# Attention scores as one 64-row product per head, into two PSUM banks, in place of one 128-row product with zero blocks

## What is computed

```
scores = scale * q @ k^T                        # per batch and head, 576 x 576
Dmat   = gamma_h ** (i - j)  where i >= j, else 0
x      = (scores * Dmat) @ v
```

## Time and profile before

| | |
|---|---|
| median of 3 runs | 727.16 us (726.26 to 732.09) |
| the profiled execution's own time | 731.02 us |
| its span, first to last instruction | 729.2 us |
| TensorE matmul busy | 669.4 us (92%), 4248 instructions |
| VectorE, ScalarE, GpSimd busy | 282.0, 220.0, 363.3 us |
| attention stage | 11.9 to 153.8 us |
| score product (L613) | 192 instructions, 50.5 us busy |

### The profile page before, as it was taken

How to read it: one execution, slowest core, us unless ns; L and a number is a source line. 1 busy time by engine, 2 the same in 40 slices (tenths; PEclk the granted TensorE clock), 3 DMA queues, 4 the chain that set the end, 5 groups by cost and what they waited for, 6 DMA issues and landing times.

```text
span 729.2 us, 14483 instructions
## 1 busy us (share of the span) xinstructions
PE 669.4 (92%) x4248; PEld 549.5 (75%) x4249; DVE 282.0 (39%) x595; ACT 220.0 (30%) x505; POOL 363.3 (50%) x226
## 2 busy tenths in 40 slices
PE   2989799953999699999999999978999999999997
PEld 1667467732778588888888888856998998898895
DVE  2456456666112233222324233334375066057031
ACT  1445355420212122222222222234434244244211
POOL 2646436404355999999999998938011002000000
PEclk9999989985899899999999999988999999999999
DMA  9999959513994434334444334332102102100101
GB/s 248 271 229 264 265 136 268 147 33 29 102 345 147 133 137 151 136 131 146 144 130 142 131 130 143 92 117 68 37 19 77 36 0 79 50 0 0 65 1 66
DMA packets 69717, 88.34 MB, mean 121 GB/s; under 512 B 14592, under 2 KB 42880, under 8 KB 69568
## 3 DMA queue, kind: packets, MB, share of 16 engines
q1 hardware_dynamic: 51264, 64.40, 30.4%
q0 software_dynamic: 3472, 11.28, 6.5%
q10 hardware_dynamic: 14944, 12.24, 5.2%
HBM read 71.89 MB, written 17.84 MB: 123 GB/s over the span
## 4 chain that ended last, share of the span: by engine, by line
PE 80%; DMA 9%; issue 4%; DVE 3%; POOL 2%; ACT 1%; POOLq 0%; ACTq 0%; DVEq 0%
PE ps L721 25%; PE ps L711 24%; DMA xg<-x_rows,slot_token 5%; PE ps L654 5%; PE ps L613 4%; PE ps L624 3%; PE ps L709 2%; PE ps L712 2%; PE ps L642 2%; PE ps L755 2%; PE ps L637 2%; PE ps L718 2%; DMA consts_sb<-constants 2%; PE ps L722 2%; DMA x_rows<-x_sb 1%
## 5 line engine op out<-in xcount | busy, mean ns | idle before, releaser
L542 POOL TENSOR_TENSOR w_lo<-stage,w_hi 128x1024 f32 x48 | 115.6, 2408 | 8.0 <-POOL w_hi L540 8.0
L540 POOL TENSOR_TENSOR w_hi<-stage,zero 128x1024 f32 x48 | 92.6, 1930 | 5.6 <-issue 5.6
L711 PE MATMUL ps<-w_lo,w_hi 128*128 128x288 f32 (+2 forms) x268 | 93.0, 347 | 0.0
L496 POOL TENSOR_TENSOR q_blocks<-q_in,consts_sb 64x576 f32<-64x576 f32 x32 | 44.8, 1401 | 70.7 <-PE ps L642 57.1
L721 PE MATMUL ps<-w_lo,xt_hi 128*128 x184 | 73.8, 401 | 0.3 <-issue 0.3
L721 PE MATMUL ps<-w_lo,ht_hi 128*128 x184 | 72.3, 393 | 0.0
L711 PE MATMUL ps<-w_hi,w_lo 128*128 128x512 f32 (+2 forms) x201 | 69.9, 348 | 0.0
L711 PE MATMUL ps<-w_hi 128*128 128x512 f32 (+2 forms) x201 | 69.8, 347 | 0.0
L1258 DVE TENSOR_TENSOR xt_lo<-ps,xt_hi 128x512 fp32r<-128x512 f32 x25 | 17.3, 691 | 126.0 <-ACT xt_hi L964 116.6
L977 ACT CAST ht_hi<-ps 128x512 fp32r<-128x512 f32 x50 | 26.9, 591 | 126.8 <-PE ps L755 117.0
L721 PE MATMUL ps<-w_hi,ht_hi 128*128 x161 | 63.2, 392 | 0.0
(11 more groups left out here) (177 smaller groups left out, 1452.4 us busy)
## 6 DMA issues: line engine op xcount, KB each, us to landing
stage<-in_w SPq DMA_DIRECT2D x64, 512.0 KB
y_slots<-y_sb ACTq DMA_DIRECT2D x25, 256.0 KB
q_in<-in_q_t SPq DMA_DIRECT2D x16, 288.0 KB, 3.6
kn_in<-in_k_n SPq DMA_DIRECT2D x16, 288.0 KB, 4.5
k_in<-in_k_t SPq DMA_DIRECT2D x16, 288.0 KB, 4.8
v_in<-in_v_n SPq DMA_DIRECT2D x16, 288.0 KB, 6.1
x_rows<-x_sb ACTq DMA_DIRECT2D x16, 288.0 KB, 4.4
out<-out_sb SPq DMA_DIRECT2D x16, 256.0 KB, 2.0
```

What stands on the lines that cost most here:

```text
L496: nc.gpsimd.tensor_tensor(q_blocks[d, u, h, :].rearrange("p (c t) -> p c t", c=NC), q_in[d, u, :].rearrange("p (c t) -> p c t", c=NC), q_d ...
L540: nc.gpsimd.tensor_tensor(hi, stage[:, j % HP, :], zero[:, 0:1].broadcast_to([P, PIECE]), ALU.add).then_inc(hi_done, 1)
L542: nc.gpsimd.tensor_tensor(lo, stage[:, j % HP, :], hi.bitcast(F32), ALU.subtract).then_inc(split_done, 1)
L711: nc.tensor.matmul(to, *p, start=False, stop=False)
```

## The change

The score product is made per head: only the head's 64 rows of `k_in` and of its plane in `q_blocks`, 96 columns each. Head 0 and head 1 write to two different banks, (0, 1) for even chunks and (6, 7) for odd ones, so there are two score buffers in place of three, and `scores` wait for the mask of c-2. The sum of the state moves from bank 6 to bank 2. The zero blocks stay, since L637 still reads them.

```diff
-        score_ps = ps[0:C, 0:3, 0:2 * C]
+        def score_ps(k):
+            low = (0, 6)[k]
+            return ps[0:C, low:low + 2, 0:C]
...
-        state_ps = ps[:, 6, 0:DH]
+        state_ps = ps[:, 2, 0:DH]
...
-                u, k = hp % 2, c % 3
+                u, k = hp % 2, c % 2
...
-                pe.wait_ge(probs_ready, n * NC + c + 1)
-                nc.tensor.matmul(score_ps[:, k, :], k_in[:, hp, c * C:(c + 1) * C],
-                                 q_blocks[:, u, :, c * C:(c + 1) * C]).then_inc(scores_ready, 1)
+                pe.wait_ge(probs_ready, n * NC + c + 2)
+                t = slice(c * C, (c + 1) * C)
+                for h, d in enumerate(heads):
+                    mm = nc.tensor.matmul(score_ps(k)[:, h, :], k_in[d, hp, t], q_blocks[d, u, h, t])
+                mm.then_inc(scores_ready, 1)
...
-                nc.vector.tensor_tensor(probs[:, c % 3, :, :], score_ps[:, c % 3, :].rearrange("p (h t) -> p h t", h=2),
+                nc.vector.tensor_tensor(probs[:, c % 3, :, :], score_ps(c % 2),
                                         inside_c[:, 2 * hp:2 * hp + 2, :], ALU.mult).then_inc(probs_ready, 1)
```

## The result

The changed kernel takes **809.92 us** (808.36 to 810.47, 4 runs) against 729.54 us before on the same chips (726.26 to 732.09, 4 runs): ratio **1.110**, 95% interval 1.104 to 1.116. I had forecast 729.1 us, with a range up to 746. The profiled execution took 809.8 us with a span of 808.0 us. The last turn product of the attention starts at 232.4 us in place of 153.8: 78.6 of the 78.8 us that the span grew lie in the attention stage.

A forecast was written before the change was run, and what follows sets the result against it. TensorE's queue was taken to bound the attention stage; 75 x 0.02 at full clock + 0.5 + 0.2 at loop starts - 5 x 0.07 in cold steps = +1.9 us, rounded to 2, on 727.16: 729.1 us, range 723 to 746.

The forecast's parts named there:

- (4): Score part of a step at the lower clock: 0.70 us against 0.77, -0.07 us on some 9 steps.
- forecast case: Whole kernel: row halves work in parallel, switch and open load cancel the saving, clock rises as before; 729.1 us, chance 72.
- rival (C): Attention steps: thinner streaming doesn't earn the full clock, +1.0 us a step; 770 or 807 us, chance 8 in 100.
- (1): Score products: 96 columns per head, both row halves at once, two pairs taking 0.17 us in place of 0.326.
- Rival (A): Score products: the heads' halves run one after the other, +17 us, 745 us; chance 12 in 100.
- (2): Before the scores: one more change of array shape, from 128 to 64 rows, costing 0.09 us of emptying a step.
- (3): Score weight load: no longer hidden under the product before, 0.08 us, two heads' loads starting some 0.01 us apart.
- Rival (B): Before the scores: no emptying between 128-row and 64-row arrays, load and switch hidden; 722 us, chance 6 in 100.
- (5): Two score buffers: the tighter mask wait costs nothing in steady steps, 0.5 and 0.2 us at the loop starts.
- (6): The rest: mask reading two banks, moved state, one more matmul a step and later stages add nothing.

The follow-up runs named there:

- warmed kernel: Changed kernel plus unread dense products in each loop pass, 18 before the first scores and 22 before those of c=2: 741.50 us, ratio 1.0175.
- hybrid: Changed kernel with the scores of the first 12 of 48 steps per loop pass as one 128-row, 192-column product: 733.42 us, ratio 1.0065.
- early-only: Changed kernel plus 36 unread dense products ahead of the loop, none inside it: 776.01 us, and 810.59 us in the second run.
- two-buffer kernel: Kernel before with only the score buffers cut from three to two, scores waiting for the mask of c-2: 733.17 us, ratio 1.0043.

## Why the prediction was wrong

**The step that failed is (4), carried into the choice between the forecast case and rival (C).** In (4) I counted some 9 steps at the lower clock, the same as before the change, with no row that says that the changed steps would earn the higher one; the runs show all 96 at it. What (4) says of one such step was right (2.32 us in place of 2.39). The price of (C) was right (2.32 us a step and 807 us; measured 2.32 and 809.9), its chance of 8 in 100 was not, and the range left it out. The argument against it was that the clock had fallen only after TensorE stood idle and never for thin streaming. That row is about *keeping* the level; I used it for *getting* it. The runs separate the two: the warmed kernel and the hybrid (dense first steps) keep the full clock through thin steps (1.345 us each), the changed kernel and, in its profiled run, the second pass of the early-only one (dense products ahead of the loop) never get it in 96 and 48 of them. Which part of the changed step withholds it, fewer columns, the added change of shape or the row halves in short pieces, the runs don't separate. The earlier trace rows also held the question: in the kernel before every rise came while it worked at the lower clock in steps of the dense form.

**(1) Half the columns, both halves at once: right.** Two pairs at the full clock take what four column halves take: in the warmed kernel two of the four instructions start at 109.75 and two 0.16 us later. Rival (A) fell; its price was added up a little high (0.18 x 75 is 13.5, the sum 744 us).

**(2) and (3) One more emptying and an open load: right.** 0.44 us forecast, 0.44 measured in the warmed kernel, +0.016 a step. The open load shows by itself in the two-buffer kernel: from 61.79 to 62.29 are 0.50 us, so 0.08 are left for it beside 0.33 of streaming and 0.09 of emptying. Rival (B) fell with the warmed kernel's rows. So even at full clock the halved product gives nothing: 0.16 us less streaming against 0.17 us of switch and load.

**(5) The tighter wait: right where it stood, and its condition too.** In the warmed changed kernel the step two after c = 4 takes the 1.345 us of the others; without the emptying, in the two-buffer kernel, the wait lay bare at 0.15 us once in six steps. The loop start, in the changed kernel:

```profile
126.03 0.67 DVE L1091 TENSOR_TENSOR probs<-ps,consts_sb 96x192 f32<-96x192 f32 x2 [3.09 <-PE ps L620]
126.43 0.40 PEld L620 LDWEIGHTS ps<-q_blocks,k_in 64*96 64x96 f32 x4 [0.47 <-DVE probs L1091]
...
127.00 0.29 PEld L631 LDWEIGHTS ps<-v_in,k_dec 96*64 96x64 f32 x4 [0.17 <-issue]
...
127.17 0.34 PEld L649 LDWEIGHTS ps<-probs,v_in 96*64 96x64 f32 x4
127.27 0.53 PE L649 MATMUL ps<-probs,v_in 96*64 96x96 f32 x4
```

The first mask ends at 126.38 and the output product starts at 127.27, 0.89 us later, where it was 0.06: +0.83, forecast 0.8.

**(6)** held for VectorE and ScalarE, which wait for TensorE as before. The hybrid, 4.7 us (3.1 to 6.5 us by its interval) over the kernel beside it, is dearer than my 2 us for the form at full clock: 72 x 0.016 = 1.2 and two starts of up to 0.8 leave some 2 us. A term that (6) left out may be in it: TensorE's jump back to the top of the loop.

```profile
88.95 2.45 PE L624 MATMUL ps<-q_blocks,k_in 128*96 128x192 f32 x6 [8.27 <-issue]
```

TensorE stood 8.27 us there, where it was 0.29 in the kernel before, and the pause from turn product to turn product was 13.8 us against 9.3.

## What to carry to other kernels

Before you shorten a product in a stretch where TensorE is the bound, ask whether the steps that remain still *earn* the full clock after each pause, and not only whether they would keep it: here 0.16 us saved per step by one product cost 1.0 us per step in all of them. The change between array shapes cost an emptying (0.09 us) and a weight load in the open (0.08 us) here at full clock; such a product has to be cut by more than that, or put beside others of its shape, which no run here tried with useful work. And where a profile's clock is 1.00 from the start, compare the durations of lines that didn't change before believing it.

## What the runs showed of the hardware

- TensorE stayed at the lower clock through 96 us of work without a gap (changed kernel, 24 to 120 us, 0.133 us an instruction), and in the early-only kernel, with 0.50 shown, while it was busy in 93.59 of 95.00 us at the same 0.133. In these two kernels being busy was not enough to be granted the full clock; the kernels with denser steps got it (rises at 24.1, 23.5 and 20.0 us in the kernel before, the hybrid and the one with six turn products, where an instruction went from 0.175, 0.161 and 0.144 us to 0.086, 0.079 and 0.090).
- Once granted, it was kept by thin steps of 1.345 us, over 48 in a row (warmed kernel, both passes), though the same steps had not earned it in 96. The 810.59 us run of the early-only kernel is the exception.
- A kernel on the border gets the level at differing moments, or keeps it in one run and not in the next: 766.77 and 783.34 us, and 776.01 and 810.59, for two runs each of one kernel.
- Where TensorE jumps back to the top of the loop it stood for 0.29 us in the kernel before. With more TensorE instructions in the body it stood longer, but not in proportion to them: 3.45 us in the changed kernel, 3.48 with the score pair nine times, 6.57 with 40 dense products, 8.27 in the hybrid. The changed kernel and the early-only one have the same loop body and stood 3.45 and 6.64 us, while the core's DMA engines were busy to a share of 0.38 and of 1.03. All that stood over 6 us did so at a share of 0.96 or more; that the transfers are the cause is not shown.
